# Tokens in two groups, the first group's expert layers between the second group's attention heads

## The chip, the cores and the metric

The kernel runs on one core of a Trainium2 chip. The metric is the device time of one execution in microseconds (us). Engines are named TensorE (PE), VectorE (DVE), ScalarE (ACT), GpSimd (POOL) and SyncE (SP, which issues DMAs here).

## The reference

Three layers in a row, in float32. Top-k attention (2 batches, 8 heads, 576 positions, head size 64), a mixture of 8 experts where each of the 1152 tokens goes to one expert, and a second layer in which each token goes through all 4 experts.

```
scores = q @ k.T / 8;  kth = 32nd largest of each row
attn = softmax(where(scores >= kth, scores, -1e9));  x = attn @ v      # tokens x 512
logits = x @ w_gate + modality_bias[modality_id];  e = argmax(logits)
x = softmax(logits)[e] * (relu(x @ w1[e]) @ w2[e])                     # 512 -> 1024 -> 512
out = sum over 4 experts of p[:, e] * (relu(x @ w1b[e]) @ w2b[e])
```

## The kernel before

Tokens lie in nine tiles of 128 rows. Float32 products are made from parts: each operand is split into a high part (rounded on ScalarE) and a low part (the difference, on VectorE or GpSimd), and `product` issues three matmuls, high by high, low by high, high by low. All PSUM is one tensor `bank` of eight banks of 512 columns.

**Attention.** A tile has eight heads, so there are 72 heads. For a head TensorE makes the scores (six matmuls of 288 columns; twelve in tile 4, which holds rows of both batches), ScalarE copies them to `sc`, VectorE finds the 32nd largest of each row with MAX8 and MATCH_REPLACE8 (two heads interleaved, `find_thresholds`), ScalarE makes the exponentials, GpSimd masks them (`mask`: compare, then multiply), TensorE transposes the result in five blocks, ScalarE copies those to `attT`, and TensorE multiplies with v (ten matmuls of 65 columns). Each engine's program has its order written out: the transposes of a head come TR_LAG = 5 heads behind its scores, the product with v AV_LAG = 6 behind. Scores alternate between banks 0, 1 and banks 2, 3; four transposed blocks lie in bank 4, the fifth beside the scores of the other parity; the products with v gather in banks 5 and 6; bank 7 serves the transposes of q, of the finished tile x, and the gate's logits. `sc` holds eight heads. Tiles run in loops on each engine.

**Routing.** After attention of all tiles, VectorE works out for each token its expert, its rank and its row in slots: a slot is 128 rows of one expert. TensorE helps with two ranks matmuls and a sum over tokens. There is room for 16 slots; how many are used depends on the data.

**First layer.** `slot(s)` gathers 128 rows of x by an indirect DMA, transposes and splits them, multiplies with w1 (24 matmuls of 512 columns), applies relu, transposes, splits, multiplies with w2 (24 matmuls) and stores the rows. Where a slot starts another expert, the weights are split on ScalarE and VectorE beforehand. Nine slots run in a loop, further ones under an If.

**Second layer.** Rows are gathered back in token order and scaled. For each expert, blocks of three tiles: `up` (8 x 12 matmuls of 384 columns), `down` (3 x 24 of 512 columns), in the order up 0, up 1, down 0, up 2, down 1, down 2.

Of the kernel before, what the change touches and what calls it, by code (L numbers as in the profile page):

```python
# [11 lines left out]
P = 128  # L25
NEG = -3.0e38


def attention_and_experts(nc, q, k, v, modality, w_gate, modality_bias, w1, w2, probs2, w1b, w2b, out, x_dram, y_dram):
# [11 lines left out]
    SLOTS = (N + E * (P - 1)) // P  # L41
# [3 lines left out]
    NBLK = T // TB  # L45
    BW = TB * P
    assert B == 2 and D == 64 and T == 2 * SPLIT + 1 and H == 8 and E == 8 and DC == 4 and FC == 8

    with ExitStack() as ctx:
# [3 lines left out]
        def sbuf(stack, name, shape, dt=F32):  # L53
            return stack.enter_context(nc.sbuf_tensor(name, shape, dt))


        ident = sbuf(ctx, "ident", [P, P])
        before = sbuf(ctx, "before", [P, P])
        ones = sbuf(ctx, "ones", [P, P])
        x_tok = sbuf(ctx, "x_tok", [P, T, DM])  # L60
        w1_raw = sbuf(ctx, "w1_raw", [P, DC, F])
        w2_raw = sbuf(ctx, "w2_raw", [P, FC, DM])
        wg = sbuf(ctx, "wg", [P, DC, E])
        mbias = sbuf(ctx, "mbias", [P, 2, E])
        mod_i = sbuf(ctx, "mod_i", [P, T, 2], I32)
        mod_f = sbuf(ctx, "mod_f", [P, 2, T])
        bias_t = sbuf(ctx, "bias_t", [P, T, E])
        pr = sbuf(ctx, "pr", [P, T, E2])
        pr_n = sbuf(ctx, "pr_n", [P, T, E2])
        pr_s = sbuf(ctx, "pr_s", [P, T])  # L70
        pr_e = sbuf(ctx, "pr_e", [P, T])
        logits = sbuf(ctx, "logits", [P, T, E])
        lg_a = sbuf(ctx, "lg_a", [P, T, E])
        lg_b = sbuf(ctx, "lg_b", [P, T, E])
        onehot = sbuf(ctx, "onehot", [P, T, E])
        tilebase = sbuf(ctx, "tilebase", [P, T + 1, E])
        lmax = sbuf(ctx, "lmax", [P, T])
        lidx = sbuf(ctx, "lidx", [P, T])
        gate_w = sbuf(ctx, "gate_w", [P, T])
        gate_s = sbuf(ctx, "gate_s", [P, T])  # L80
        ecol = sbuf(ctx, "ecol", [P, E])
        ecol_i = sbuf(ctx, "ecol_i", [P, E], I32)
        jcol = sbuf(ctx, "jcol", [P, SLOTS + 1])
        jcol_i = sbuf(ctx, "jcol_i", [P, SLOTS + 1], I32)
        bcol = sbuf(ctx, "bcol", [P, P])
        bcol_i = sbuf(ctx, "bcol_i", [P, P], I32)
# [1186 lines left out]
```

## Time and profile before

| | |
|---|---|
| times of three runs | 1026.86, 1027.62, 1033.14 us (median 1027.62) |
| profiled execution: its span | 1026.1 us |
| TensorE, VectorE, ScalarE, GpSimd busy | 92%, 55%, 31%, 27% of the span |
| mean granted TensorE clock | 0.814 of full speed |
| DMA moved | 51.91 MB |

The span runs from the first to the last instruction of one execution; the times of whole runs have a little more around it. A busy share is an average over stages with different limits. The granted clock is what the chip allowed TensorE, as a share of 2.4 GHz; it has two levels, 0.50 and 1.00, and a stretch shows their mean.

### The profile page before, as it was taken

The page shows a single profiled execution, that of the slowest core. Times are in us where ns is not written, and L with a number is a line of the kernel's source. Part 1 is how long each engine was busy: PE and PEld are TensorE (multiplying, and loading weights), DVE is VectorE, ACT ScalarE, POOL GpSimd, SP SyncE. Part 2 cuts the span into 40 slices and gives each one's busy share as a digit, 9 for nine tenths or more (in the row PEclk, how much of TensorE's full clock was granted, in tenths as well). Part 3 has the DMA queues.
Part 4 walks back from the last instruction along what each step waited for, and adds up shares of the span by engine and source line. Part 5 has one row for each costly group of instructions (what it writes and reads, how often), then busy time and mean ns, then how long its engine had stood idle before and what let it go on. Part 6 is the DMA issues. An engine that isn't in the chain of part 4 may idle for free.

```text
span 1026.1 us, 14239 instructions
## 1 busy us (share of the span) xinstructions
PE 945.9 (92%) x4525; PEld 825.8 (80%) x4526; DVE 567.7 (55%) x1118; ACT 322.9 (31%) x640; POOL 280.7 (27%) x233
## 2 busy tenths in 40 slices
PE   4599999999899999839899958999999999999998
PEld 3488888887788888727777748998999899989897
DVE  6899999869998879266224243323422241414121
ACT  3344544436434444135233242211212031303010
POOL 7566666545566555010111122000000000000000
PEclk8565665759755555559999987999999999999999
DMA  9300000000000000059115116002200220000001
GB/s 179 110 2 20 1 21 20 1 21 1 21 1 20 10 0 11 11 181 343 60 41 204 41 42 236 1 1 82 82 1 1 82 82 0 0 0 0 20 20 51
DMA packets 40054, 51.91 MB, mean 51 GB/s; under 512 B 23888, under 2 KB 23888, under 8 KB 40016
## 3 DMA queue, kind: packets, MB, share of 16 engines
q1 hardware_dynamic: 33120, 38.80, 11.6%
q0 software_dynamic: 3888, 12.59, 4.1%
q10 hardware_dynamic: 3008, 0.05, 0.2%
q8 instruction: 19, 0.31, 0.1%
q14 instruction: 19, 0.16, 0.0%
HBM read 42.00 MB, written 9.44 MB: 50 GB/s over the span
## 4 chain that ended last, share of the span: by engine, by line
PE 83%; issue 6%; DVE 5%; DMA 3%; ACT 1%; POOL 1%; POOLq 0%; ACTq 0%; DVEq 0%
PE bank L1004 21%; PE bank L1006 19%; PE bank L1005 19%; PE bank L1047 12%; PE bank L1026 5%; PE bank L991 4%; PE bank L1027 1%; DMA y_dram<-ys 1%; PE bank L1060 1%; DVE top L735 1%; DVE work L731 1%; DMA xs_raw<-x_dram,tok_cur 1%; DMA pr<-in_moe_domain_probs_dram 0%; DVE top L723 0%; DVE kTl L694 0%
## 5 line engine op out<-in xcount | busy, mean ns | idle before, releaser
L412 POOL TENSOR_SCALAR keep<-sc,top 128x576 f32<-128x576 f32 x70 | 120.5, 1721 | 124.4 <-DVE top L735 111.2
L1047 PEld LDWEIGHTS bank<-v_one,attT 128*128 128x128 f32 (+2 forms) x680 | 136.0, 287 | 20.8 <-issue 13.3
L735 DVE MAX8 top<-work 128x8 f32<-128x576 f32 x216 | 152.3, 746 | 0.0
L1047 PE MATMUL bank<-v_one,attT 128*128 128x65 f32 (+2 forms) x680 | 152.2, 386 | 0.0
L1004 PE MATMUL bank<-xTh,w1h 128*128 128x384 f32 x384 | 129.6, 338 | 1.6 <-DVE xTl L938 1.6
L1005 PE MATMUL bank<-xTh,w1l 128*128 128x384 f32 x384 | 129.3, 337 | 0.0
L1006 PE MATMUL bank<-xTl,w1h 128*128 128x384 f32 x384 | 129.3, 337 | 0.0
L944 DVE SCALAR_TENSOR_TENSOR hTl<-bank,hTh 128x384 fp32r<-128x384 f32 x96 | 52.9, 556 | 133.8 <-ACT hTh L656 133.4
L656 ACT ACTIVATE hTh<-bank 128x384 fp32r<-128x384 f32 x96 | 46.9, 491 | 212.1 <-PE bank L1006 212.1
L1006 PE MATMUL bank<-w2l,hTh 128*128 128x512 f32 x288 | 112.2, 390 | 0.0
L1005 PE MATMUL bank<-w2h,hTl 128*128 128x512 f32 x288 | 112.2, 390 | 0.0
L1004 PE MATMUL bank<-w2h,hTh 128*128 128x512 f32 x288 | 112.0, 389 | 0.0
L417 POOL TENSOR_TENSOR att<-keep,ex 128x576 f32<-128x576 f32 x70 | 98.7, 1410 | 26.8 <-PE bank L1027 21.9
L731 DVE MATCH_REPLACE8 work<-top,work 128x576 f32<-128x576 f32 x144 | 105.8, 742 | 0.1
L512 ACT ACTIVATE sc<-bank 128x576 f32<-128x576 f32 x72 | 46.7, 650 | 174.4 <-PE bank L1006 174.0
L955 DVE SCALAR_TENSOR_TENSOR x_tok<-bank,pr_e,x_tok 128x512 f32<-128x512 f32 x27 | 20.3, 750 | 115.0 <-PE bank L1006 115.0
L1026 PE MATMUL bank<-ident,att 128*128 128x128 f32 x288 | 71.4, 395 | 11.0 <-ACT attT L530 6.9
L1004 PEld LDWEIGHTS bank<-xTh,w1h 128*128 128x128 f32 x384 | 72.9, 190 | 2.2 <-issue 2.0
L1004 PE MATMUL bank<-kTh,qTh 64*128 64x288 f32 x160 | 72.2, 453 | 2.4 <-DVE kTl L694 1.9
L1005 PEld LDWEIGHTS bank<-xTh,w1l 128*128 128x128 f32 x384 | 72.8, 190 | 0.3
L1006 PEld LDWEIGHTS bank<-xTl,w1h 128*128 128x128 f32 x384 | 72.8, 190 | 0.0
L723 DVE MAX8 top<-sc 128x8 f32<-128x576 f32 x72 | 52.8, 750 | 31.1 <-ACT sc L512 30.7
(170 smaller groups left out, 1519.5 us busy)
## 6 DMA issues: line engine op xcount, KB each, us to landing
w_raw<-in_moe_w_dram SPq DMA_DIRECT2D x56, 512.0 KB, 5.5
y_dram<-ys POOLq DMA_DIRECT2D x11, 256.0 KB, 2.3
q_raw<-in_q_dram SPq DMA_DIRECT2D x18, 128.0 KB, 2.6
v_one<-in_v_dram POOLq DMA_DIRECT2D x18, 128.0 KB, 7.8
x_dram<-x_cur SPq DMA_DIRECT2D x9, 256.0 KB, 2.1
out_dram<-x_tok SPq DMA_DIRECT2D x9, 256.0 KB, 2.0
x_tok<-in_k_dram SPq DMA_DIRECT2D x8, 256.0 KB, 6.1
y_dram<-zero POOLq DMA_DIRECT2D x1, 1792.0 KB, 10.0
```

The source lines that it names most:

```text
L412: nc.gpsimd.tensor_scalar(keep[:, :], sc[:, i, :], top8[:, r, 3, 7:8], None, ALU.is_ge).then_inc(keep_made, 1)
L417: nc.gpsimd.tensor_tensor(att[:, i % 2, :], keep[:, :], ex[:, r, :], ALU.mult).then_inc(att_made, 1)
L656: nc.scalar.activation(hTh[:, b % 2, f, :], bank[:, HB + f % 4, 0:BW], ACT.Relu).then_inc(h_high, 1)
L723: nc.vector.max(out=top8[:, h % 4, 0, :], in_=sc[:, h, :]).then_inc(max_found, 1)
L731: nc.vector.match_replace(out=work[:, j, :], in_to_replace=top8[:, h % 4, i, :], in_values=sc[:, h, :] if i == 0 else work[:, j, :], imm_v ...
L735: nxt = nc.vector.max(out=top8[:, h % 4, i + 1, :], in_=work[:, j, :])
L944: nc.vector.scalar_tensor_tensor(out=hTl[:, b % 2, f, :], in0=bank[:, HB + f % 4, 0:BW], scalar=0.0, in1=hTh[:, b % 2, f, :].bitcast(F32), ...
L1004: nc.tensor.matmul(dst, high_lhs, high_rhs, start=start, stop=False)
L1005: nc.tensor.matmul(dst, low_lhs, high_rhs, start=False, stop=False)
L1006: return nc.tensor.matmul(dst, high_lhs, low_rhs, start=False, stop=stop)
L1026: nc.tensor.transpose(bank[:, ATB, c * P:(c + 1) * P], att[:, r, c * P:(c + 1) * P], ident[:, :])
L1047: last = nc.tensor.matmul(bank[r0:r0 + nr, AVB + half, o:o + D + 1], attT[0:kk, r, c, r0:r0 + nr], v_one[0:kk, b * H + h, c, :], start=(c ...
```

## The change

The nine tiles form group a (tiles 0 to 2) and group b (tiles 3 to 8), each with its own routing, slots and second layer; a has room for 10 slots. The attention loops are written out as steps p = 0 to 80 on every engine. In step p TensorE makes the scores of head p, the product with v of head p-6 and the transposes of head p-5, then what the generator `beside` gives for this step, then the turns for x and q.

Attention now has banks 0 to 3: scores in 0 and 1 for every head, one bank (TBK = 2) in which the transposes of att, x and q take turns, and bank 3 for one head's product with v and the logits, copied out per head by ScalarE (`copy_av`). The fifth transposed block lies in bank 0 beside the scores. `sc` holds four heads, `mask` writes its comparison into `att`. In tile 4 the product with v runs once for each batch's rows. Banks 4 to 7 belong to the work beside.

Group a's routing runs in steps 33 on. Its slots run in steps 39 to 63, four steps a slot (up half 0, up half 1, two turns, with the last slot's two down halves): five slots always, five more under an If at step 64, whose Else counts the semaphores up. GpSimd makes the low parts of x and h from copies that ScalarE writes to SBUF. Its second layer begins in step 69, one block of 8 up and 3 down uses for each of four experts, and goes on after the last head, with group b's routing between. Then group b's slots and second layer run in the loops of before, with six tiles. SyncE stores group a's rows before it loads group b's second expert of the first layer.

```diff
+class Group:
+    def __init__(self, name, first, tiles, experts):
+        self.name, self.first, self.tiles = name, first, tiles
+        most = (tiles * P + experts * (P - 1)) // P
+        self.slots = most + most % 2
...
+    GA, GB = Group("a", 0, TB, E), Group("b", TB, T - TB, E)
+    NBLK = GB.tiles // TB
...
-        SCB, ATB, AVB, XB = 0, 4, 5, 7
-        LAST = (HS, HS + P)
-        EXP_LAG, TR_LAG, AV_LAG = 2, 5, 6
-        ROUND_AT = 3
...
+        SB, TBK, AVB, MB = 0, 2, 3, 4
+        LAST, LGT = HS, P
+        EXP_LAG, TR_LAG, AV_LAG, X_LAG, L_LAG = 2, 5, 6, 15, 16
+        STEPS = (T - 1) * H + L_LAG + 1
+        A_START, SPREAD, A_RARE, A_PASS = 39, 5, 64, 69
+        A_USES = FC + TB
+        HB, HTB, YB, XB = 0, 2, 4, 7
...
+        def q_at(p):
+
+            t, r = p // H + 1, p % H
+            late = t in (SPLIT, SPLIT + 1)
+            high = t if t < T and r == (H - 1 if late else H - 2) else None
+            low = t if t < T and r == H - 1 else None
+            return high, low
...
+            def take_turn(kind, i):
+                if turn_use[kind, i] > 1:
+                    pe.wait_ge(turn_read, turn_use[kind, i] - 1)
...
+            def transpose_att(g):
+                pe.wait_ge(att_made, g + 1)
+                take_turn("att", g)
+                pe.wait_ge(sc_copied, min(g + TR_LAG + 1, HEADS))
+                for c in range(KC - 1):
+                    nc.tensor.transpose(bank[:, TBK, c * P:(c + 1) * P], att[:, g % 2, c * P:(c + 1) * P], ident[:, :])
+                nc.tensor.transpose(bank[0:KL, SB, LAST:LAST + P], att[:, g % 2, (KC - 1) * P:S], ident[:, :]).then_inc(turn_made, 1)
...
+            def scores(g):
+                t, h = g // H, g % H
                 pp = slice(D * (h % 2), D * (h % 2) + D)
+                segs = [(t % 2, 0 if t < SPLIT else 1)] if t != SPLIT else [(0, 0), (1, 1)]
+                if h == 0:
+                    pe.wait_ge(turn_read, turn_use["ql", t])
+                if g > TR_LAG:
+                    pe.wait_ge(turn_read, turn_use["att", g - TR_LAG - 1])
+                elif g >= 1:
+                    pe.wait_ge(sc_copied, g)
                 for i in range(2):
+                    cols = slice(i * HS, (i + 1) * HS)
+                    for j, (r, b) in enumerate(segs):
+                        last = product(bank[:, SB + i, 0:HS], qTh[pp, r, h // 2, :], qTl[pp, r, h // 2, :],
+                                       kTh[b][pp, h // 2, cols], kTl[b][pp, h // 2, cols], j == 0, j == len(segs) - 1)
...
+            def att_times_v(g):
+                t, h = g // H, g % H
+                if g >= 1:
+                    pe.wait_ge(av_copied, g)
+                if x_at(g + AV_LAG - 1, L_LAG) is not None:
+                    pe.wait_ge(lg_read, x_at(g + AV_LAG - 1, L_LAG) + 1)
+                pe.wait_ge(turn_read, turn_use["att", g])
+                rows = [(0, P, 0 if t < SPLIT else 1)] if t != SPLIT else [(0, CUT, 0), (CUT, P, 1)]
+                for r0, r1, b in rows:
                     for c in range(KC):
                         kk = P if c < KC - 1 else KL
...
+            def a_up(s, i):
+                if i == 0:
+                    pe.wait_ge(a_xs_split, s + 1)
+                    if s >= 1:
+                        pe.wait_ge(a_relu, 2 * (s - 1) + 1)
+                elif s >= 1:
+                    pe.wait_ge(a_hT_copied, 2 * s)
+                for c in range(DC):
+                    if i == 0:
+                        pe.wait_ge(aw1_split, s * DC + c + 1)
+                    ff = slice(i * 512, (i + 1) * 512)
+                    last = product(bank[:, MB + i, :], xsTh[:, s % 2, c, :], xsTl[:, s % 2, c, :], w1h[:, c, ff], w1l[:, c, ff], c == 0, c == DC - 1)
+                last.then_inc(a_h, 1)
...
+            def a_down(s, i):
+                pe.wait_ge(a_hs_split, 2 * s + i + 1)
+                if i == 0 and s >= 1:
+                    pe.wait_ge(a_ys, s)
+                for f in range(4 * i, 4 * i + 4):
+                    if f % 2 == 0:
+                        pe.wait_ge(aw2_split, s * DC + f // 2 + 1)
+                    last = product(bank[:, MB + 3, :], hsTh[:, f, :], hsTl[:, f, :], w2h[:, f, :], w2l[:, f, :], f == 0, f == FC - 1)
+                last.then_inc(a_d, 1)
...
+                yield from clock.until(A_START - 2)
+                a_x(0)
+                for s in range(SPREAD + 1):
+                    at = A_START + 4 * s
+                    yield from clock.until(at)
+                    if s < SPREAD:
+                        a_up(s, 0)
+                    if s + 1 < SPREAD:
+                        a_x(s + 1)
+                    yield from clock.until(at + 1)
+                    if s < SPREAD:
+                        a_up(s, 1)
+                    for i in range(2):
+                        yield from clock.until(at + 2 + i)
+                        if s < SPREAD:
+                            a_turn(s, i)
+                        if s >= 1:
+                            a_down(s - 1, i)
+                yield from clock.until(A_RARE)
+                for s in range(SPREAD, GA.slots):
+                    with pe.If(guarded(pe, GA, s)):
...
+                    with pe.Else():
+                        pe.drain().then_inc(a_xT_made, 1)
+                        pe.drain().then_inc(a_h, 2)
+                        pe.drain().then_inc(a_hT_made, 2)
+                        pe.drain().then_inc(a_d, 2)
...
+                for e in range(E2):
+                    for f in range(FC):
+                        n = e * A_USES + f
+                        yield from clock.until(A_PASS + n)
+                        if n >= 4:
+                            pe.wait_ge(a2_done, n - 3)
+                        for c in range(DC):
+                            if f == 0:
+                                pe.wait_ge(aw1_split, (GA.slots + e) * DC + c + 1)
+                            last = product(bank[:, a_bank(n), 0:BW], w1h[:, c, f * P:(f + 1) * P], w1l[:, c, f * P:(f + 1) * P],
+                                           xTh_a[:, c, :], xTl_a[:, c, :], c == 0, c == DC - 1)
+                        last.then_inc(a2_made, 1)
+                    for t in range(TB):
+                        n = e * A_USES + FC + t
+                        yield from clock.until(A_PASS + n)
+                        pe.wait_ge(a2_done, max(e * A_USES + FC, n - 3))
+                        o = t * P
+                        for f in range(FC):
+                            if t == 0 and f % 2 == 0:
+                                pe.wait_ge(aw2_split, (GA.slots + e) * DC + f // 2 + 1)
+                            last = product(bank[:, a_bank(n), :], hTh_a[:, f, o:o + P], hTl_a[:, f, o:o + P], w2h[:, f, :], w2l[:, f, :], f == 0, f == FC - 1)
+                        last.then_inc(a2_made, 1)
...
+            for p in range(STEPS):
+                clock.now = p
+                if p == SPLIT * H:
+                if p < HEADS:
+                    scores(p)
+                if 2 <= p < 2 + T - 1 - SPLIT:
+                    key_transposes(SPLIT - 1 + p)
+                if p == AV_LAG:
+                    pe.wait_ge(v_ones, B)
+                    pe.wait_ge(v_loaded, 16 * (B * H + B))
+                if 0 <= p - AV_LAG < HEADS:
+                    att_times_v(p - AV_LAG)
+                if 0 <= p - TR_LAG < HEADS:
+                    transpose_att(p - TR_LAG)
+                advance(work_beside)
+                if x_at(p, X_LAG) is not None:
+                    x_transpose(x_at(p, X_LAG))
+                high, low = q_at(p)
+                if high is not None:
+                    q_transposes(high, "qh")
+                if low is not None:
+                    q_transposes(low, "ql")
+                if x_at(p, L_LAG) is not None:
+                    x_logits(x_at(p, L_LAG))
+            for p in range(STEPS, STEPS + 3):
+                clock.now = p
+                advance(work_beside)
+            ranks(GB)
+            for p in range(STEPS + 3, STEPS + 7):
+                clock.now = p
+                advance(work_beside)
+            sum_tokens(GB)
+            clock.now = 1000
...
+            def copy_attT(g):
+                act.wait_ge(turn_made, turn_use["att", g])
+                if g >= 2:
+                    act.wait_ge(av_made, g - 1)
+                nc.scalar.activation(attT[:, g % 2, 0:KC - 1, :].rearrange("p c q -> p (c q)"), bank[:, TBK, :], ACT.Copy)
+                nc.scalar.activation(attT[0:KL, g % 2, KC - 1, :], bank[0:KL, SB, LAST:LAST + P], ACT.Copy).then_inc(turn_read, 1)
+
+            def copy_av(g):
+                t, h = g // H, g % H
+                act.wait_ge(av_made, g + 1)
+                if h == 0 and t >= 2:
+                    act.wait_ge(x_ready, t - 1)
+                nc.scalar.activation(av[:, t % 2, h, :], bank[:, AVB, 0:W], ACT.Copy).then_inc(av_copied, 1)
...
+            def a_highs_of_slot(s, which, done):
+                with act.If(starts_expert(act, s)):
+                    which(s, range(DC))
+                with act.Else():
+                    act.drain().then_inc(done, DC)
...
+                for s in range(1, SPREAD + 1):
+                    yield from clock.until(A_START + 4 * s)
+                    if s >= 2:
+                        a_copy_y(s - 2)
+                    if s < SPREAD:
+                        a_lows_of_slot(s, a_low1, aw1_split)
+                    yield from clock.until(A_START + 4 * s + 2)
+                    if s >= 2:
+                        a_lows_of_slot(s - 1, a_low2, aw2_split)
+                yield from clock.until(A_START + 4 * SPREAD + 4)
...
+            for i, _ in enumerate(routing):
+                clock.now = STEPS + (3 if i < 5 else 7)
+                advance(work_beside, 2)
+            clock.now = 1000
+            for _ in work_beside:
...
             split_low(0, w1_raw, w1h, w1l, w1_high, w1_split)
+            split_low(0, w2_raw, w2h, w2l, w2_high, w2_split)
             slot_xT_low(1)
-            split_low(0, w2_raw, w2h, w2l, w2_high, w2_split)
...
             load_kth(0)
+            for t in range(TB):
+                sp.wait_ge(a2_done, (E2 - 1) * A_USES + FC + t + 1)
+                sp.dma_start(out[t * P:(t + 1) * P, :], x_tok_a[:, t, :]).then_inc(stored, 16)
```

## Rows read from the trace of the kernel before

**Rows 1.** The page: busy us, share of the span, instructions.
```profile
PE 945.9 (92%) x4525; PEld 825.8 (80%) x4526; DVE 567.7 (55%) x1118; ACT 322.9 (31%) x640; POOL 280.7 (27%) x233
```

**Rows 2.** Stretches: length; PE, PEld, DVE, ACT, POOL busy; clock; DMA share; GB/s.
```profile
51.50:228.00 176.50, 174.12 (x798) 148.77 (x797) 162.28 (x350) 79.76 (x185) 109.73 (x71) 0.62 0.05 13
...
310.00:358.00 48.00, 48.00 (x190) 41.25 (x190) 41.74 (x90) 20.00 (x47) 28.71 (x20) 0.50 0.05 16
...
406.00:434.50 28.50, 25.95 (x111) 23.27 (x110) 10.71 (x26) 7.04 (x18) 2.86 (x2) 0.50 0.03 10
434.50:456.90 22.40, 4.30 (x17) 3.63 (x17) 16.22 (x54) 5.09 (x6) 2.21 (x4) 0.50 0.37 120
```

**Rows 3.** Timeline of one head, low clock: start, us, instruction.
```profile
337.53 0.61 PE L1004 MATMUL bank<-kTh,qTh 64*128 64x288 f32 x1
...
339.26 2.59 PE L1047 MATMUL bank<-v_one,attT 128*128 128x65 f32 x10
...
340.83 0.58 ACT L529 ACTIVATE attT<-bank 128x512 f32<-128x512 f32 x1
...
341.30 0.26 ACT L530 ACTIVATE attT<-bank 64x128 f32<-64x128 f32 x1
...
341.78 1.12 PE L1026 MATMUL bank<-ident,att 128*128 128x128 f32 x4
...
342.69 0.42 PE L1027 MATMUL bank<-ident,att 128*64 128x128 f32 x1
...
343.04 0.60 PE L1004 MATMUL bank<-kTh,qTh 64*128 64x288 f32 x1
```

**Rows 4.** Timeline of one head, high clock.
```profile
244.74 0.39 PE L1004 MATMUL bank<-kTh,qTh 64*128 64x288 f32 x1
...
247.76 0.26 ACT L530 ACTIVATE attT<-bank 64x128 f32<-64x128 f32 x1
...
248.16 0.63 PE L1026 MATMUL bank<-ident,att 128*128 128x128 f32 x4 [0.86 <-ACT attT L530]
...
248.83 0.39 PE L1004 MATMUL bank<-kTh,qTh 64*128 64x288 f32 x1
```

**Rows 5.** VectorE's groups of instructions: count | busy us, mean ns | idle before.
```profile
L735 DVE MAX8 top<-work 128x8 f32<-128x576 f32 x216 | 152.3, 746 | 0.0
L731 DVE MATCH_REPLACE8 work<-top,work 128x576 f32<-128x576 f32 x144 | 105.8, 742 | 0.1
...
L723 DVE MAX8 top<-sc 128x8 f32<-128x576 f32 x72 | 52.8, 750 | 31.1 <-ACT sc L512 30.7
...
L885 DVE TENSOR_TENSOR w1l<-w_raw,w1h 128x1024 fp32r<-128x1024 f32 x28 | 32.5, 1219 | 4.8 <-ACT w1h L596 3.4 <-issue 1.4
```

**Rows 6.** A stretch of five us in attention.
```profile
105.00:110.00 5.00, 4.71 (x35) 3.91 (x34) 5.00 (x11) 3.57 (x9) 4.63 (x3) 1.00 0.00 2
110.00:115.00 5.00, 5.00 (x26) 4.27 (x25) 5.00 (x11) 2.04 (x7) 1.99 (x3) 0.62 0.00 0
```

**Rows 7.** Stretches: one slot, the change over, one expert of the second layer.
```profile
507.30:520.50 13.20, 12.59 (x61) 10.28 (x60) 2.66 (x5) 2.76 (x6) 1.80 (x4) 1.00 0.12 40
...
605.50:621.70 16.20, 3.09 (x12) 2.17 (x13) 13.32 (x16) 5.68 (x8) 9.78 (x9) 0.62 0.37 109
621.70:722.00 100.30, 100.29 (x512) 92.41 (x513) 29.89 (x48) 18.65 (x34) 2.13 (x2) 0.98 0.20 72
```

**Rows 8.** Timeline of matmuls of 512 columns, three apart, at either clock.
```profile
460.94 0.63 PE L1004 MATMUL bank<-w1h,xsTh 128*128 128x512 f32 x1
...
462.22 0.63 PE L1004 MATMUL bank<-w1h,xsTh 128*128 128x512 f32 x1
...
474.26 0.39 PE L1004 MATMUL bank<-w1h,xsTh 128*128 128x512 f32 x1
...
474.94 0.39 PE L1004 MATMUL bank<-w1h,xsTh 128*128 128x512 f32 x1
```

**Rows 9.** A register load from a tile on VectorE: ns min/median/max.
```profile
L900 DVEq TENSOR_LOAD <-by_slot_i x10: 302/307/312, 467.7 to 587.4; - x10
```

More of the change, by code:

```diff
@@ new lines, in _ @@
+            work_beside = beside()
+            for g in range(HEADS - 2):
+                mask(g)
+                if g == 2:
+                    store_zeros(y_a, SPREAD, GA.slots)
+                if g == 4:
+                    store_zeros(y_dram, GB.tiles, GB.slots)
+                if g % H == 0 and g // H + 1 < T:
+                    split_q(g // H + 1)
+                clock.now = g + 4
+                advance(work_beside)
+            clock.now = 1000
+            for _ in work_beside:
+                pass
@@ new lines, in a_lows_of_slot, with a_copy_y @@
+            def a_lows_of_slot(s, which, done):
+                with dve.If(starts_expert(dve, s)):
+                    for c in range(DC):
+                        which(s, c)
+                with dve.Else():
+                    dve.drain().then_inc(done, DC)
+            def a_copy_y(s):
+                dve.wait_ge(a_d, 2 * s + 2)
+                if s >= 1:
+                    dve.wait_ge(a_stored, 16 * s)
+                nc.vector.tensor_copy(ys[:, :], bank[:, MB + 3, :]).then_inc(a_ys, 1)
@@ new lines, in _ @@
+            work_beside = beside()
+            for g0 in range(0, HEADS, 2):
+                clock.now = g0 + 3
+                between = ()
+                if g0 >= AV_LAG + 6 and (g0 - AV_LAG - 6) % H == 0:
+                    between = normalise((g0 - AV_LAG - 6) // H)
+                find_thresholds(g0, between, work_beside)
+                if g0 < 4:
+                    for t in range(SPLIT + 1 + g0, SPLIT + 3 + g0):
+                        key_low(t)
+            for g in range(HEADS - 2, HEADS):
+                dve.wait_ge(thr_found, HEADS)
@@ new lines, in sum_tokens, with a_x @@
+            def sum_tokens(g):
+                pe.wait_ge(g.places_made, 2)
+                for t in range(g.tiles):
+                    last = nc.tensor.matmul(bank[:, g.token_bank, 0:g.slots], g.row_hot[:, t, :], g.slot_token[:, t, :], start=(t == 0), stop=(t == g.tiles - 1))
+                last.then_inc(g.tokens_summed, 1)
+            def a_x(s):
+                pe.wait_ge(a_xs_loaded, 16 * (s + 1))
+                if s == 1:
+                    pe.wait_ge(a_xT_copied, 1)
+                elif s >= 2:
+                    pe.wait_ge(a_hT_copied, 2 * (s - 2) + 1 if s < SPREAD else 2 * (s - 1) + 1)
+                transposes(MB + 2, lambda c: xs_raw[:, c * P:(c + 1) * P]).then_inc(a_xT_made, 1)
```

1541 lines of the change are left out of this document (929 added, 612 removed).

## Prediction

> **What bounds the kernel now.** I read the page's line of busy times first: TensorE 945.9 of 1026.1 us, VectorE 567.7, ScalarE 322.9, GpSimd 280.7 [rows 1]. TensorE is the bound on average, but an average over stages, so the table by stretches comes next [rows 2]. Attention runs from about 16 to 434 us. In the stretch 310 to 358 (one tile, eight heads) TensorE is busy 48.00 of 48.00 us and its granted clock is 0.50, the lower level (1.2 GHz), while VectorE has 41.74 us. From 51.5 to 228 it is 174.12 of 176.5 us at 0.62. So attention has no idle TensorE time to fill; it has a slow TensorE. The idle time lies behind it: 434.5 to 456.9, where the routing runs, has 4.30 us of work in 22.40.
>
> The timeline gives one head at the low clock [rows 3]: scores start at 337.53, probabilities times values at 339.26, the five transposes at 341.78, the next head's scores at 343.04, so 5.51 us: 1.73 + 2.52 + 1.26. At the high clock [rows 4] the same round is 248.83 - 244.74 = 4.09 us, of which 0.86 is a wait for ScalarE's copy of the transposed block; the work is 3.2. VectorE's work for a head is four MAX8 of 0.75 and three MATCH_REPLACE8 of 0.74; their busy times add up to 363.8 us for 72 heads (MAX8 152.3 and 52.8, second and third replace 105.8, the first half of that, 52.9), 5.05 a head [rows 5]. That is the floor of a head when the clock is high. The clock does come up for some 10 us at a time, as at 105 to 110 (1.00) [rows 6].
>
> The later stages: a slot (one 128-row pass through an expert of the first layer) takes 13.1 us at clock 1.00, the change over from slots to the second layer 16.2, one expert of the second layer over nine tiles 100.3 [rows 7].
>
> **Work counted, not time.** Computing the gate from the reference's inputs gives 11 slots before. By groups it is 5 (three experts: 1, 2 and 2 slots) for tokens 0 to 383, and 7 (1, 3, 3) for the rest. The change therefore adds a slot, and loads and splits seven more weight pairs. SPREAD is 5, so all slots of group a run between heads and the five guarded ones take their Else.
>
> **1. Steps 7 to 38, attention alone.** This is where I expect the loss. Before, scores alternate between two pairs of banks. Now there is one pair, and the last transpose block of head p-5 lies in its columns 288 to 415; scores(p+1) waits for that block's copy. PE's order in a step is scores, values, transposes, so the transposes, ScalarE's copy and the next scores come in series. The copy takes 0.58 and then 0.26 us, overlapping to 0.73 (340.83 to 341.56) [rows 3]; from its end to TensorE's next start 0.14 (248.02 to 248.16) [rows 4], and 0.07 of the modelled tail of the last transpose. The bubble is 0.94 us; bounds: 0 (if ScalarE's end were hidden by weight loads) and 1.2. The step is 5.51 + 0.94 = 6.45 us. The other copy, that of the scores, lies under the values' 2.52 us and costs nothing.
> The shared transpose bank adds at each tile's end: q high 1.0 us (four of five transposes in 1.26), then x and q low each 1.0 + 0.58 + 0.17, since every turn waits for the copy of the last; with the logits some 0.9, that is 5.4 us a tile.
> Sum: head 7's scores start near 51.5 as before (the first stretch [rows 2] was cut there; the fill waits for VectorE and the loads of v). Then 32 x 6.45 = 206; three tile ends and a smaller one, 20; seven heads of the mixed tile with six more score matmuls (1.73 - 0.29 = 1.44), 10; VectorE waits in order for the logits of tile 2 when it begins group a's routing in step 33, and its masks come late, 4 (0 to 10). Step 39 starts at 291.5. Before, it started near 223 (the 40th of 72 heads).
>
> The Trainium skill (TensorE: Matmul & The Clock Gate, What's actually happening) says that the gate gives the full clock to an array that is kept busy. The trace disagrees in the plain form of that rule: 48.00 of 48.00 us busy stayed at 0.50 [rows 2].
>
> **2. Steps 39 to 63, slots of group a between heads.** Each step adds 12 matmuls of 512 columns, four transposes, and in one of four steps four more. The same matmuls cost 0.427 us at the low clock ((462.22 - 460.94) / 3) and 0.227 at the high one ((474.94 - 474.26) / 3) [rows 8]. A step is then 3.2 + 12 x 0.227 + 0.45 = 6.4 us at the high clock, and the bubble vanishes under the added work; 25 steps 160, tile ends 12, the mixed tile's values in row halves 4: 176. At the low clock it is 5.51 + 5.12 + 1.0 = 11.6, so 291 + 20 = 311. VectorE has 25 x 5.05 = 126, six splits of 4 x 1.22 [rows 5] = 29, ys copies and normalising 8, and some eight register loads with branches (0.31 us for the load [rows 9], about 1 with its surroundings, an estimate): 171. Two engines so close together, with ScalarE's four splits in a row ahead of its copies in the same step, don't overlap fully. I take 190, near the high-clock end, because in the slot stage this stream of matmuls came from 0.50 to 1.00 and held it [rows 7, 8].
>
> **3. Steps 64 to 68.** Five heads with the clock falling back, 31 us, and the five Else blocks of each engine (load, branch, drains), 5 (2 to 10, from the same 0.31): 36.
>
> **4. Steps 69 to 77.** The last heads beside eight up blocks and one down block: nine steps near 6.3, set by VectorE's thresholds plus splits, and one tile end: 58. It ends at 575.5.
>
> **5. The rest of group a's second layer.** One expert over nine tiles is 100.3 us [rows 7], so one over three is 33; four are 132, of which 22 are done in part 4. Left 110; the routing of group b, its ranks and token sums lie beside it and cost 5 in waits. This is the real gain: before, the tail and the routing from 406 to 456.9 had 30.25 us of TensorE work in 50.9 [rows 2].
>
> **6. Change over to group b.** VectorE adds the last block (0.75), then splits w1 (4.9), w2 (4.9) and x (0.7) in order before the first matmul; w1's high part is ready, its low part not, as VectorE is held by the second layer. 11 us, and 3 for a start at the low clock (the first 24 matmuls at 0.427 in part): 14 (8 to 18).
>
> **7. Group b.** Seven slots 92 and 2 for the first switch; change over 16; second layer of six tiles 4 x 66.9 = 267; last add and store 3. Its loops keep their form, and the six down blocks still cover the w1 splits.
>
> Sum: 291.5 + 190 + 36 + 58 + 110 + 5 + 14 + 94 + 16 + 267 + 3 = 1084.5 us, and 1.5 for what lies outside the span (1027.62, the median of three runs, less 1026.1). The forecast is 1086 us, 5.7% slower.
>
> **The rivals.**
> (a) The clock comes up at each tile's end, as at 105 us [rows 6]. Before, the 33 heads from 51.5 to 228 took 176.5 us, where 33 at the pace of 310 to 358 (48 / 8 = 6.0) would take 198, so bursts saved 21. With the same saving here, the stage of slots at 170 and the small terms at their lower ends: 270.5 + 170 + 30 + 50 + 108 + 2 + 11 + 92 + 16 + 267 + 3 = 1019.5, so 1021, no change. Against it: the turns stand apart by a copy now, so the transposes are less dense, and from 310 to 434 even the dense form raised nothing [rows 2]. Chance 0.10.
> (b) Faster: the interleaved dense matmuls and the denser mix bring the full clock to the whole of attention. It decides when steps 7 to 38 take under 5.5 us each; heads then run at VectorE's 5.05: 51.5 + 32 x 5.1 + 4 = 219 in place of 270.5 above, so 969. This is what a plain reading of the busy rule would give. The Trainium skill's rule (TensorE: Matmul & The Clock Gate, What's actually happening) is that reading; the stretch at 0.50 speaks against it [rows 2]. Chance 0.05.
> (c) The matmuls of group a don't hold the clock between heads: part 2 costs up to 311, half of the way 250. 1146 to 1207. For it: attention alone drops the clock after some 10 us [rows 6]; against it, a 2.7 us block comes in each step. 0.15.
> (d) The banks cost nothing (the copy hidden): 32 x 0.94 = 30 less, 1056. Still slower, since filling a TensorE that is already full saves nothing. 0.12.
> (e) My sum as it stands, 1065 to 1115: 0.58.
>
> **How the numbers follow.** The time is that of (e). The range leaves out (b) and the end of (c): 1010 to 1160. One per cent is about what a measurement can tell from no change. Faster by over 1%: (b), the better half of (a) and some of what I don't see, 0.12; within it: 0.08; slower: 0.80.
>
> **What would show it.** Steps before 39: heads at 6.4 to 6.5 us with a gap of about 0.9 us in front of each first score matmul, released by ScalarE's attT copy, and clock 0.50; head 39 at 291. Between heads: clock over 0.85 and 7.6 us a step. A TensorE full from 575 to 690; then a gap of 11 us whose waits end with VectorE's split of x. Wrong if the clock before step 39 is above 0.65, or below 0.75 from 39 to 63, or if the guarded blocks cost tens of us.

## The result, and the profile after

The changed kernel takes 1226.7 us (median of 4 runs, 1225.6 to 1227.3) against 1030.4 (4 runs, 1026.9 to 1042.8): a ratio of 1.194, 95% interval 1.189 to 1.199. The forecast was 1086, with a range up to 1160. The ratio is formed without one slower run of the kernel before (1042.8), and against the median of its other three, 1027.6, the loss is 199 us. The direction was right; a loss of 58 was forecast.

The page of the changed kernel, busy line:
```profile
PE 998.5 (81%) x4649; PEld 854.6 (70%) x4650; DVE 637.8 (52%) x1165; ACT 405.7 (33%) x790; POOL 305.2 (25%) x246
```
TensorE has 52.6 us more work than before [rows 1] in a span 199.5 us longer (1225.6): 147 us are new idle time on the engine that bounded the kernel before. The stretches (columns as in [rows 2]) are cut at the forecast's parts:
```profile
51.50:231.00 179.50, 152.33 (x580) 125.66 (x581) 123.14 (x253) 71.18 (x171) 83.67 (x55) 1.00 0.07 22
231.00:314.70 83.70, 55.86 (x235) 49.46 (x233) 53.87 (x129) 22.68 (x51) 25.91 (x18) 1.00 0.16 57
314.70:574.00 259.30, 185.36 (x952) 151.29 (x950) 151.09 (x276) 107.99 (x226) 107.77 (x71) 0.77 0.14 48
574.00:622.70 48.70, 30.48 (x128) 26.03 (x129) 26.32 (x48) 16.35 (x35) 17.69 (x12) 0.57 0.30 105
622.70:690.00 67.30, 49.67 (x255) 46.06 (x254) 42.86 (x82) 23.31 (x56) 14.26 (x10) 0.75 0.03 11
690.00:811.00 121.00, 113.69 (x548) 100.77 (x549) 56.81 (x104) 40.45 (x55) 1.23 (x2) 0.96 0.38 140
811.00:828.00 17.00, 12.55 (x56) 9.66 (x54) 6.01 (x7) 4.38 (x5) 2.05 (x2) 0.95 0.12 47
828.00:926.00 98.00, 86.13 (x396) 69.60 (x397) 40.79 (x48) 34.12 (x51) 10.50 (x18) 0.94 0.46 163
926.00:950.00 24.00, 9.14 (x36) 6.57 (x36) 13.45 (x16) 9.56 (x12) 8.52 (x7) 0.70 0.52 197
950.00:1225.00 275.00, 271.33 (x1356) 244.64 (x1356) 84.79 (x122) 55.36 (x92) 0.00 (x0) 0.99 0.11 41
```
Row by row against the forecast: step 39 begins at 314.7 (291.5 forecast); steps 39 to 63 take 259.3 (190); 64 to 68, 48.7 (36); the rest of attention and of group a's second layer 188.3 (58 + 110 + 5); the change over 17 (14); group b 98, 24 and 275.6 to the end of the span (94, 16, 270). The excess is 23 + 69 + 13 + 15 + 3 + 18 = 141 us. (The cut at 314.7 lies a little inside step 39: its first score matmul starts at 310.57. By that start the excess is 19 us before the step and 73 in steps 39 to 63; the sum is the same.) In the third row no engine is full: TensorE idles 74 us of 259, VectorE 108. So the stage is set by waits between engines, and not by the work of one of them.

Attention alone, timeline of one head (compare [rows 3]):
```profile
133.85 0.61 PE L1458 MATMUL bank<-kTh,qTh 64*128 64x288 f32 x1 [0.84 <-ACT attT L788]
...
135.58 2.58 PE L1514 MATMUL bank<-v_one,attT 128*128 128x65 f32 x10
...
138.10 1.11 PE L1483 MATMUL bank<-ident,att 128*128 128x128 f32 x4
...
139.01 0.42 PE L1484 MATMUL bank<-ident,att 128*64 128x128 f32 x1
...
140.27 0.61 PE L1458 MATMUL bank<-kTh,qTh 64*128 64x288 f32 x1 [0.84 <-ACT attT L788]
```
A head is 6.42 us, with 0.84 us of wait for the copy of the transposed block: the forecast had 6.45.

Now the stalls. Waits of VectorE in steps 39 to 63 (316.6 to 575.8, between the copies of the scores of heads 39 and 64); us in total, times, longest:
```profile
DVE ys L1237 <- PE bank L1460: 51.9, 5, 11.4
DVE w2l L1218 <- ACT w2h L808: 45.2, 4, 18.0
DVE w1l L1218 <- ACT w1h L808: 6.9, 1, 6.9
```
VectorE stands 104 us in front of group a's work (ys are the copies of a slot's result, w1l and w2l the low parts of its weights), and hardly at all in front of attention's. What this does to the others is one timeline (start, us, instruction, idle before and its releaser):
```profile
420.71 5.78 DVE L1218 TENSOR_TENSOR w2l<-w2r,w2h 128x1024 fp32r<-128x1024 f32 x4 [11.84 <-ACT w2h L808]
...
434.92 1.72 POOL L630 TENSOR_SCALAR att<-sc,top 128x576 f32<-128x576 f32 x1 [11.79 <-DVE top L1104]
...
438.21 0.65 ACT L772 ACTIVATE sc<-bank 128x576 f32<-128x576 f32 x1 [9.33 <-POOL att L633]
...
439.01 1.09 PE L1483 MATMUL bank<-ident,att 128*128 128x128 f32 x4 [6.68 <-ACT sc L772]
```
Read it from the top. VectorE stood 11.84 us for the high part of w2, split it, and only then took up the thresholds queued behind it. So GpSimd's mask waited 11.79 us; so the copy of later scores into one of four buffers waited 9.33 for a mask to free it; so TensorE waited 6.68, since its transposes need that copy to have left the columns they write. The row names the copy of the scores as what TensorE waits for; the cause is four links back.

In steps 32 to 38 (231 to 315) the same engine waits in the first group's routing and, in the last row, in front of the first slot's w1:
```profile
DVE logits L1142 <- ACT logits L803: 20.7, 1, 20.7
...
DVE a_tok_i L1205 <- PE bank L1539: 9.5, 1, 9.5
DVE w1l L1218 <- ACT w1h L808: 9.5, 2, 5.9
```

### The profile page after: what moved, and what is told of

The parts are those of the page before. It is cut to its first block, busy times and chain, and to the rows that moved or that the text cites. A ratio compares the mean times of both kernels' runs of the same rounds, so it can differ in the third digit from the quotient of the medians.

```text
span 1225.6 us, 13824 instructions
## 1 busy us (share of the span) xinstructions
PE 998.5 (81%) x4649; PEld 854.6 (70%) x4650; DVE 637.8 (52%) x1165; ACT 405.7 (33%) x790; POOL 305.2 (25%) x246
## 4 chain that ended last, share of the span: by engine, by line
PE 68%; issue 13%; DVE 7%; POOL 4%; ACT 4%; DMA 3%; SPq 0%; DVEq 0%; POOLq 0%; ACTq 0%
PE bank L1458 17%; PE bank L1459 15%; PE bank L1460 15%; PE bank L1514 10%; PE bank L1483 5%; PE bank L1453 3%; POOL att L630 2%; DVE work L1099 2%; POOL att L633 2%; DVE top L1104 2%; DMA y_dram<-b_ys 1%; PE bank L1484 1%; DVE w2l L1350 1%; PE bank L1527 1%; ACT sc L772 1%
## 5 line engine op out<-in xcount | busy, mean ns | idle before, releaser
L630 POOL TENSOR_SCALAR att<-sc,top 128x576 f32<-128x576 f32 x70 | 120.5, 1722 | 364.0 <-DVE top L1104 188.3
L1514 PE MATMUL bank<-v_one,attT 128*128 128x65 f32 (+3 forms) x800 | 159.4, 358 | 1.6 <-issue 1.6
L1514 PEld LDWEIGHTS bank<-v_one,attT 128*128 128x128 f32 (+3 forms) x800 | 139.4, 257 | 26.1 <-issue 17.4
L1483 PEld LDWEIGHTS bank<-ident,att 128*128 128x128 f32 x288 | 46.4, 199 | 97.9 <-POOL att L633 86.1
L633 POOL TENSOR_TENSOR att<-att,ex 128x576 f32<-128x576 f32 x70 | 101.6, 1451 | 5.8
L1459 PE MATMUL bank<-xTh,w1l 128*128 128x384 f32 x256 | 86.9, 340 | 0.0
L1458 PEld LDWEIGHTS bank<-kTh,qTh 64*128 64x128 f32 x160 | 43.8, 274 | 59.8 <-ACT attT L788 35.7
L787 ACT ACTIVATE attT<-bank 128x512 f32<-128x512 f32 x72 | 43.0, 597 | 73.8 <-PE bank L1484 73.8
L1459 PE MATMUL bank<-kTh,qTl 64*128 64x288 f32 x160 | 63.4, 396 | 0.0
L1460 PE MATMUL bank<-kTl,qTh 64*128 64x288 f32 x160 | 63.3, 396 | 0.0
```

What stands on the lines that cost most here:

```text
L630: nc.gpsimd.tensor_scalar(att[:, g % 2, :], sc[:, g % 4, :], top8[:, g % 4, 3, 7:8], None, ALU.is_ge).then_inc(keep_made, 1)
L633: nc.gpsimd.tensor_tensor(att[:, g % 2, :], att[:, g % 2, :], ex[:, g % 3, :], ALU.mult).then_inc(att_made, 1)
L787: nc.scalar.activation(attT[:, g % 2, 0:KC - 1, :].rearrange("p c q -> p (c q)"), bank[:, TBK, :], ACT.Copy)
L1458: nc.tensor.matmul(dst, high_lhs, high_rhs, start=start, stop=False)
L1459: nc.tensor.matmul(dst, low_lhs, high_rhs, start=False, stop=False)
L1460: return nc.tensor.matmul(dst, high_lhs, low_rhs, start=False, stop=stop)
```

## The experiments

Theory T1: VectorE's work beside attention is placed by a step counter (`clock.now = g0 + 3`) that says when VectorE *issues* it. VectorE then stands at waits for things that TensorE and ScalarE do later, with the thresholds of coming heads behind. Rivals are named where they were tested. The kernel before, run beside the variants, ranged from 1011.8 to 1050.6 over the four groups of runs; the changed kernel was not run again beside them, but the first 31 heads of all kernels with the same code agree within 1.5 us. So the variants are compared with each other by their times and stretches, and ratios to before carry their intervals.

| kernel | us | ratio to before | step 39 at | steps 39 to 63 | 64 to 68 |
|---|---|---|---|---|---|
| changed | 1226.7 | 1.194 (1.189–1.199) | 316.6 | 259.2 | 48.8 |
| late_dve | 1103.1 | 1.074 (1.067–1.080) | 291.3 | 190.2 | 40.4 |
| slots_late | 1129.5 | 1.110 (1.084–1.137) | 316.7 | 189.2 | 39.3 |
| y_late | 1202.1 | 1.147 (1.136–1.158) | 316.6 | 237.1 | 48.9 |
| w2_late | 1207.0 | 1.152 (1.136–1.167) | 316.5 | 240.5 | 49.2 |
| yw2_late | 1187.9 | 1.154 (1.121–1.188) | 316.4 | 223.1 | 48.7 |
| last_avb | 1201.9 | 1.170 (1.164–1.176) | 299.1 | 252.8 | 46.9 |
| late_last | 1085.7 | 1.067 (1.041–1.094) | 276.0 | 187.7 | 39.0 |
| noguard | 1217.7 | 1.185 (1.179–1.192) | 316.5 | 259.4 | 41.6 |
| combo | 1079.2 | 1.061 (1.035–1.087) | 276.0 | 190.2 | 32.1 |
| all_late | 1085.9 | 1.036 (1.026–1.046) | 276.0 | 186.2 | 38.4 |
| serial | 1251.3 | 1.218 (1.214–1.222) | 304.6 | 185.3 | 33.8 |
| serial_late | 1235.7 | 1.215 (1.187–1.243) | 288.9 | 185.3 | 33.8 |

(The last three columns are differences between the starts of the copies of scores of heads 39, 64 and 69 in the timelines, a little off the stretches above. The scores' first matmuls start earlier than their copies, in step 39 at 310.57 in the changed kernel and at 285.74 in late_dve. In the two serial kernels steps 39 to 68 hold attention alone.)

**late_dve**: VectorE takes all work beside one pair of heads later.
```diff
-                clock.now = g0 + 3
+                clock.now = g0 + 1
```


> VectorE runs its group a work one pair of heads later (its step counter is g0 + 1 in place of g0 + 3). Theory 1 (VectorE reaches group a's waits before TensorE and ScalarE have done their part, its thresholds stand behind them, and with four score buffers the masks, the score copies and TensorE's transposes stand too): the waits of VectorE for the down halves and for w2's high parts, 97 us in steps 39 to 63, fall below 40, the stage falls from 259 to about 205 us, the routing stretch from 84 to about 72, the whole from 1227 to about 1160. Theory 2 (the stage is long because its matmuls run at the low clock and its work is what it is): no change within 10 us, or longer, since TensorE now waits for the splits.

1103.1 us: 124 less than the changed kernel, from one number, and more than T1 had expected. Its stretches up to head 69:
```profile
228.00:291.30 63.30, 58.80 (x250) 52.00 (x248) 47.61 (x113) 24.19 (x55) 28.32 (x18) 1.00 0.24 84
291.30:481.50 190.20, 170.40 (x948) 139.68 (x947) 157.61 (x289) 108.11 (x227) 110.09 (x70) 0.88 0.19 65
481.50:521.90 40.40, 29.91 (x135) 25.55 (x135) 24.57 (x46) 17.99 (x39) 20.09 (x13) 0.58 0.35 126
```
The same program but for the place of VectorE's work in its queue, and the stage takes 190 us in place of 259. Of these 69, 54 are idle time of TensorE that is gone (20 us in place of 74) and 15 are shorter matmuls (170.4 us busy for 185.4), at a granted clock of 0.88 for 0.77. Theory 2 had no change or a loss.

**slots_late**: the same, but only from step 37 on, so that routing keeps its early place.
```diff
-                clock.now = g0 + 3
+                clock.now = g0 + (3 if g0 < A_START - 2 else 1)
```


> The changed kernel with VectorE's work beside two steps later only from step 37 on: routing of the first group keeps its early place. T1: the 124 us of late_dve split as the losses did against the forecast, 23 in routing before step 39 and the rest in the slots: 1103 + 23 = 1126, range 1115 to 1140, step 39 still at 314 us. T2 (most of it is in routing, whose end sets when the slots can start): 1180 or more.

1129.5: within T1's range. 97 us lie in the slots and behind them, 26 in front of them. VectorE's waits from 315 to 510 us are now
```profile
DVE top L1090 <- ACT sc L772: 20.0, 10, 6.6
DVE w2l L1218 <- ACT w2h L808: 8.8, 3, 4.6
DVE ys L1237 <- PE bank L1460: 3.8, 4, 1.7
```
12.6 us in front of group a's work in place of 104; what is left on top is VectorE's wait for the next scores of TensorE, which was there in attention alone too (60.1 us in steps 39 to 63 of serial).

**y_late, w2_late, yw2_late**: one kind of wait moved alone, then both.
```diff
                 for s in range(1, SPREAD + 1):
                     yield from clock.until(A_START + 4 * s)
-                    if s >= 2:
-                        a_copy_y(s - 2)
                     if s < SPREAD:
                         a_lows_of_slot(s, a_low1, aw1_split)
                     yield from clock.until(A_START + 4 * s + 2)
                     if s >= 2:
+                        a_copy_y(s - 2)
                         a_lows_of_slot(s - 1, a_low2, aw2_split)
```
(w2_late leaves the copy and asks for `A_START + 4 * s + 4` ahead of the last line; yw2_late has both.)

> The changed kernel with only VectorE's copies of the slots' results (ys) taken two steps later; everything else of the work beside stays where it is. Of the 97 us that slots_late gained over the changed kernel, theory T1 (each wait in VectorE's queue costs about what VectorE idles in it) puts 45 to 52 here, the idle before the ys copies between 315 and 576 us: 1175 to 1182. Rival T3 (one early wait is worth nothing alone: VectorE stands at the next, the low parts of w2, instead): 1207 or more.

> The changed kernel with only VectorE's low parts of the second weights (w2l) of a slot two steps later. T1: VectorE idled 45 us before them between 315 and 576 us, so 1182 (1175 to 1190). T3 (one wait alone is worth little): 1207 or more.

> Both edits of y_late and w2_late in one kernel (the first slot's w2l stays early, as in w2_late). In those two the time fell by what all of VectorE's waits between 315 and 576 us fell by (104 us to 80 and to 85), not by the wait that was moved. T1 in that form: left are about 26 us of w2l, 14 of w1l and 14 of ys, so 104 - 54 = 50 below the changed kernel: 1177 (1168 to 1185), near the plain sum of the two, 1182. Rival T5 (each of the two hides behind the other, so that both together give most of the 97 us of slots_late): 1130 to 1155.

25, 20 and 39 us gained. y_late fell between the theories (T1 had up to 1182 and T3 from 1207), w2_late at T3's edge: T1 as it was put, a wait moved for a wait saved, missed both. The third gave a little less than the plain sum (44), 3 us outside T1's range and far from T5. Waits of the three kernels in steps 39 to 63, y_late:
```profile
DVE w2l L1218 <- ACT w2h L808: 51.7, 4, 18.4
DVE ys L1237 <- PE bank L1459: 14.4, 2, 13.7
DVE w1l L1218 <- ACT w1h L808: 13.8, 2, 6.9
```
w2_late:
```profile
DVE ys L1237 <- PE bank L1460: 52.5, 5, 11.5
DVE w2l L1218 <- ACT w2h L808: 26.1, 4, 18.1
DVE w1l L1218 <- ACT w1h L808: 6.9, 1, 6.9
```
yw2_late:
```profile
DVE w2l L1218 <- ACT w2h L808: 29.7, 4, 17.8
DVE w1l L1218 <- ACT w1h L808: 19.3, 2, 12.4
DVE ys L1237 <- PE bank L1461: 14.0, 3, 12.9
```
y_late took 37.5 us of wait away from ys, and 6.9 came back at w1l and 6.5 at w2l: VectorE, still too early, stood at the next wait instead. Against the sum of the three waits (104.0, 85.5, 79.9, 63.0 and 12.6 us for the changed kernel, w2_late, y_late, yw2_late and slots_late) the stage took 259.2, 240.5, 237.1, 223.1 and 189.2: 70 us less for 91 us less of waiting, 0.77 us of time for each us, and the three between lie 4 to 5 us below that line. In these five kernels the stage follows the sum of the waits, and not the one that was moved.

**last_avb**: the fifth transposed block goes to the bank of the weighted sums, so that scores no longer wait for its copy and transposes no longer wait for the scores' copy.
```diff
-        LAST, LGT = HS, P
+        LAST, LGT = 2 * P, P
...
-                pe.wait_ge(sc_copied, min(g + TR_LAG + 1, HEADS))
...
-                nc.tensor.transpose(bank[0:KL, SB, LAST:LAST + P], ...)
+                if g >= 1:
+                    pe.wait_ge(av_copied, g)
+                nc.tensor.transpose(bank[0:KL, AVB, LAST:LAST + P], ...)
...
-                if g > TR_LAG:
-                    pe.wait_ge(turn_read, turn_use["att", g - TR_LAG - 1])
-                elif g >= 1:
+                if g >= 1:
                     pe.wait_ge(sc_copied, g)
```


> The fifth transposed block moves from the scores' bank to the bank of the product with v, so scores wait only for the copy of the last scores. If the bubble in front of the scores is the bank's: steps 8 to 31 fall from 6.42 to about 5.5 us, 22 us in all, and with steps 64 to 71 the whole falls to about 1200. Rival: the loop transposes, mask on GpSimd, copy of the scores, transposes is the bound of a step: it measures about 5.3 us, so it would stop the fall at 5.3 to 5.6 and cost nothing; if it is longer than it looks, steps stay at 6.4 and the time at 1227.

1201.9, 25 less, as expected. Two heads of it:
```profile
126.84 0.61 PE L1458 MATMUL bank<-kTh,qTh 64*128 64x288 f32 x1
...
132.00 0.42 PE L1485 MATMUL bank<-ident,att 128*64 128x128 f32 x1
132.35 0.61 PE L1458 MATMUL bank<-kTh,qTh 64*128 64x288 f32 x1
```
A head is 5.51 us, that of [rows 3] to the hundredth, with no wait left. So the price of the single pair of score banks was the place of one block, 0.91 us a head (0.94 forecast). The loop over GpSimd's mask, the rival of the expectation, had its bound at 5.3 to 5.6 and is not ruled out as the next limit. A whole tile, heads 16 to 24, fell from 56.8 to 53.5 us (172.6 - 115.8, 162.9 - 109.4), less than eight times that: the ends of tiles got longer. Steps 39 to 63 still take 252.8 us. TensorE's transposes no longer wait for the copy of the scores there, but for ScalarE's copy of the product with v (43.4 us in all), which stands in ScalarE's queue behind that copy. So the stall doesn't need the shared bank; it found another last link.

**late_last**: late_dve and last_avb together. 

> The two edits that helped singly, together: VectorE takes the work beside two steps later (alone 1103), and the fifth transposed block of a head lies in the bank of the weighted sums, so that scores wait for the copy of the scores only (alone 1202, 25 below the changed kernel). Theory T1 (two waits in different places, one in a queue, one in the bank cycle): the gains add, 1103 - 25 = 1078, range 1065 to 1088, attention alone 5.5 us a head, 6 us or more between tiles. Rival T2 (once the queue's waits are gone another engine sets the step): 1095 to 1105, with steps between heads 40 and 63 still at 7.4 us or more.

1085.7, within the range of T1: 17 on top of late_dve, 8 less than if the gains added in full.

**noguard**: the guarded slots and the tests for a new expert are left out, the answers of this data written in.
```diff
-                with dve.If(starts_expert(dve, s)):
-                    for c in range(DC):
-                        which(s, c)
-                with dve.Else():
-                    dve.drain().then_inc(done, DC)
+                if s in (1, 3):
+                    for c in range(DC):
+                        which(s, c)
+                else:
+                    dve.drain().then_inc(done, DC)
```
(and so on ScalarE and SyncE; the loops over `range(SPREAD, GA.slots)` are gone.)

> Leaves out group a's five guarded slots (never taken with these inputs) and replaces its tests of whether a slot starts another expert by what these inputs give. Theory 1: step 64 falls by about 10 us, the stage of slots by 5 to 10, the whole to about 1210. Rival (branches stall every engine and are the main cost of the stage): the stage of slots falls by 40 us or more, the whole below 1180.

1217.7: 9 us, of which 7 lie in steps 64 to 68 (48.8 to 41.6), where the Else blocks stood. The forecast had 5 (2 to 10) for them. The stage of slots did not fall (259.4), so the tests and branches in it were not its cost, and the rival is out.

**combo**: late_last with noguard. 

> The two edits of late_last, and the guarded slots and the tests of whether a slot starts an expert left out (this data's answers written in), which alone gave 9. T1: 1078 - 9 = 1069, range 1055 to 1080: still above the kernel before (1028), because attention alone is slower per head than before and nothing in these edits touches that. T2: 1090 or more.

1079.2: 6.5 less than late_last, 7 of them again in steps 64 to 68. It is the fastest version found, and still 6% slower than before (3.5 to 8.7%), and 2.7% slower than even the slowest run of the kernel before (1050.6).

**all_late**: late_last with the copies of ys two steps later still. 

> late_last (1086) with the copies of the slots' results another two steps later. VectorE no longer stands long at them there, so T1 expects 1083 to 1090, no change; if the ys copies still hold the queue, 1060 to 1075. Both stay above the kernel before.

1085.9, no change: once VectorE no longer stands there (3.3 us in late_last), more delay buys nothing.

**serial, serial_late**: group a's layers behind the last head, with the counter as in the changed kernel and one pair later.
```diff
-        A_START, SPREAD, A_RARE, A_PASS = 39, 5, 64, 69
+        A_START, SPREAD, A_RARE, A_PASS = 139, 5, 164, 169
```


> Group a's slots and second layer all run after the last head (start steps shifted by 100); its routing stays in step 33. Theory 1 (the interleaving loses in waits about what it hides): 64 steps at 6.42 and 5.4 us a tile end put the last head near 540, then slots 75 to 90, change over 18, second layer 135, then group b's 415: about 1205, level with the changed kernel or below. Theory 2 (the interleaving pays, and the loss is in the banks and the doubled work): 1260 or more.

> The serial order (the first group's expert layers after the last head, alone 1251) with VectorE's work beside two steps later. It is the base against which the placing between heads is judged. T1 (the waits stand in routing and slots; only routing is left between heads here): 1251 - 23 = 1228, range 1215 to 1240, so that placing between heads, once mended, is worth 1228 - 1103 = 125 us. T2 (late_dve gained by the attention steps themselves, not by the work beside): 1251 - 100 or so, 1130 to 1160.

serial, at 1251.3, fell between its two theories (1205 and 1260 or more), near the second; serial_late, at 1235.7, within T1's range. Placing the layers between heads gained 1251.3 - 1226.7 = 25 us as it was written, and 1235.7 - 1103.1 = 133 with the waits mended. The idea of the change is worth 133 us against its own serial form. It loses to before because that serial form stands some 200 us above: 117 of them are there by the last head (the scores of head 71 are copied at 520.5 in serial_late and 403.8 before), the rest comes behind, where one slot and seven weight pairs were added. How those 200 divide further was tried only for the banks.

Two things can be read from the traces without a run. First, steps 39 to 63 take 185.3 us in serial_late with attention alone and 190.2 in late_dve with the five slots between: the slots are nearly free there, for the matmuls run faster. In late_dve, 91 of the 150 gaps from one score matmul of 288 columns to the next instruction of TensorE are about 0.13 us (the high level), in serial_late none is. Second, attention before had such gaps too: 63 of 246 from 51.5 to 228 us, in the first two or three heads of a tile; in the changed kernel there is none before 314 us. Heads 16 to 24 took 40.8 us before, where a whole tile at the low clock takes 48 [rows 2], and 56.8 in the changed kernel: 7 us a tile lost with the clock, beside the 7 (eight times 0.91) of the block. Why the clock no longer rises there stays open.

## Why the prediction was wrong, point by point

**The step that failed** is the price of waits in VectorE's queue, in parts 1 and 2. Part 1 gave routing "4 (0 to 10)" for masks that come late; the runs show 25 to 26 in front of step 39 (late_dve against slots_late: step 39 at 291.3 and 316.7, 1103.1 and 1129.5). Some 16 of these are routing's own (serial_late 288.9, serial 304.6); the other 10 match the 9.5 us in which VectorE stood before the first slot's w1, which has no term in the sum. Part 2 took VectorE's *busy* time of 171 us, added 19 for imperfect overlap, and never asked at which moment VectorE reaches each of group a's instructions: 70 us (slots_late). I had written for part 1 that VectorE "waits in order for the logits", so the mechanism was seen once and then not carried to the splits and to ys. What was needed stood in the changed kernel's code: `g0 + 3` against the steps at which ScalarE makes the high parts and TensorE the last matmul of a slot. With four score buffers, of eight before, a wait of about 11 us then reached TensorE; that more buffers would have held it back is not shown, as no run changed their number.

**The rest of the sum stands.** In late_dve the scores of step 39 start at 285.7 (291.5 forecast) and are copied at 291.3, steps 39 to 63 take 190.2 between copies and 193.9 between first score matmuls (190), steps 64 to 68, 40.4 (36). So part 2's 190 was the right size of a stage without the queue's waits, and the 69 us above it come with these waits. That it came out so near is partly luck: the 19 us over VectorE's 171 were a guess, and TensorE, not VectorE, is the fuller engine there (170.4 busy against 157.6). Its clock was 0.88 (over 0.85 forecast); with the stalls it was 0.77.

**Part 3**: 48.7 for 36; 9 us are the queue again (39.3 in slots_late), 7 the Else blocks (5 forecast).

**Parts 4 to 6**: 205.3 us from 622.7 to the first slot of group b, for 187. In late_dve that is about 185 (the first relu of group b's slots at 716.4, less the 11.8 by which it follows the start of the slots in the changed kernel, is 704.6; head 69 is copied at 521.9, and in the changed kernel its step starts 2 us ahead of the copy). The wait at the change over was foreseen; the row of waits from 828 to 926 us has it, with the split of x as its end (11 forecast):
```profile
PE bank L1458 <- DVE b_xsTl L1355: 9.8, 1, 9.8
```

**Part 7**, group b: 397.6 for 380 in the changed kernel, about 399.5 in late_dve. This mis-sizing is apart from the queue: 4 in the slots, 8 in their change over, 5.6 in the second layer. No run was made on it, and its cause stays open.

**The rivals.** (a) and (b), clock gains in attention, did not show: heads ran at the low clock's pace (below). (c), the interleaved matmuls don't hold the clock: in the changed kernel the stage is long and at 0.77, as (c) has it, but the clock followed the stalls: moving VectorE's work brought both 0.88 and 190 us. The spacing bears the two clocks out: of the 240 matmuls of 512 columns in the stage, 170 in late_dve and 141 in the changed kernel were followed within 0.28 us, and 38 and 59 by the 0.43 us of the low level [rows 8]. The clock's part in the 69 us is the 15 of shorter matmuls. (d), the banks cost nothing, is refuted by the 0.84 us wait and by last_avb. None of the cases held a wait that travels round four engines.

In sum, 1226.7 = 1103.1 + 123.6 for the queue's waits; of the 1103.1, 1086 was forecast. The 17 left are about group b's excess (19.5 in the profiled run, which was 2.7 us longer than the median); the other parts' differences, from -2 to +4, cancel.

## What to carry to other kernels

When work is woven into another loop, cost it twice: once by the busy time of each engine, and once by position, asking for every added wait when its engine issues it, when the thing waited for is made, and what of the other loop is queued behind. If an engine waits before work that feeds the bottleneck, delaying that work by a step may be worth more than any instruction removed; look for a stretch in which no engine is full. And a chain of waits is to be followed back past the name in the bottleneck's row, here four links.

## What the runs showed that I had not expected

The clock in the rows can't be read alone. The stretches of the changed kernel up to 314.7 us stand at 1.00, and the prediction had named a clock above 0.65 there as a sign of being wrong. Two kernels settle it. The same tile of eight heads, first in serial, then in serial_late:
```profile
376.30:433.10 56.80, 49.26 (x189) 40.86 (x189) 40.24 (x83) 22.32 (x53) 26.27 (x17) 0.50 0.04 11
```
```profile
360.60:417.40 56.80, 49.26 (x189) 40.87 (x189) 40.25 (x83) 22.34 (x54) 26.27 (x17) 1.00 0.04 11
```
Equal time, equal busy time, and a granted clock of 0.50 in one and 1.00 in the other. The spacing of matmuls decides; in serial_late, inside that tile:
```profile
386.13 0.44 PE L1459 MATMUL bank<-kTh,qTl 64*128 64x288 f32 x1
386.37 0.44 PE L1460 MATMUL bank<-kTl,qTh 64*128 64x288 f32 x1
```
0.24 us for 288 columns is one column a cycle at 1.2 GHz, the lower level; the heads up to 314 us in the changed kernel have the same 0.24. The Trainium skill (TensorE: Matmul & The Clock Gate, Wait — 56ns, not 53.3ns?) gives the same spacing, columns over 1.2 GHz, for a cold array, and its section Seeing it yourself warns that the recorded events of the gate can be unreliable; by both, the trace agrees. The same holds for whole runs: two executions of late_dve, of 1105.8 and 1100.4 us, have mean granted clocks of 0.940 and 0.814, the lower one in the shorter run. But the 1.00 of [rows 6] was real; in it the same matmuls of the kernel before stand 0.13 us apart:
```profile
108.27 0.29 PE L1004 MATMUL bank<-kTh,qTh 64*128 64x288 f32 x1
108.40 0.29 PE L1005 MATMUL bank<-kTh,qTl 64*128 64x288 f32 x1
```
